# The opening of an attention and two-MoE kernel: one product on GpSimd, the bonus pairs on ScalarE's queue, the way back in another order

## The reference

```python
for t in range(S):                                   # attention
    cur = einsum('bhd,bhe->bhde', u * k[t], v[t])    # bonus of the own step
    y[t] = einsum('bhd,bhde->bhe', r[t], state + cur)
    state = w * state + einsum('bhd,bhe->bhde', k[t], v[t])
h = x @ w_in                                         # dense layer
g = where(h > 0, h, exp(min(h, 0)) - 1)
x = g @ w_out
# experts: argmax of x @ w_gate, relu(x @ w1[e]) @ w2[e] times the gate, 384 slots each
```

## Time and profile before

| | us |
|---|---|
| median of 3 runs | 416.25 |
| lowest and highest | 415.97, 416.66 |
| profiled execution, device time | 416.52 |
| its span in the trace | 414.7 |
| TensorE busy | 406.5 (98%) |
| VectorE busy | 242.7 (59%) |
| GpSimd busy | 231.8 (56%) |
| ScalarE busy | 188.4 (45%) |

### The profile page before, as it was taken

One profiled execution on the slowest core, in us unless ns is written; L12 is line 12 of the kernel. 1 busy time (PEld: TensorE's weight loads), 2 busy tenths in 40 slices (PEclk: granted clock), 3 DMA queues, 4 the chain that ended last, 5 costly groups with the idle time before them and its releaser, 6 DMA issues.

```text
span 414.7 us, 9451 instructions
## 1 busy us (share of the span) xinstructions
PE 406.5 (98%) x3697; PEld 390.2 (94%) x3697; DVE 242.7 (59%) x576; ACT 188.4 (45%) x409; POOL 231.8 (56%) x239
## 2 busy tenths in 40 slices
PE   8999999999999999999999999999999999999994
PEld 8799799999999999999999999999999999999994
DVE  7787955375576547654754487775645546365421
ACT  4786543233433333333333555553645446464420
POOL 3789865467856685668234336075174461835531
PEclk9999999999999999999999999999999999999999
DMA  7999996204030403020018001827283844729000
GB/s 261 403 395 365 350 366 245 91 29 155 4 119 2 138 21 118 3 85 21 2 21 342 2 2 39 324 77 256 116 321 101 326 169 193 295 90 357 5 31 28
DMA packets 18650, 64.98 MB, mean 157 GB/s; under 512 B 2203, under 2 KB 11717, under 8 KB 16432
## 3 DMA queue, kind: packets, MB, share of 16 engines
q1 hardware_dynamic: 16816, 59.68, 39.5%
q0 software_dynamic: 1792, 4.73, 3.0%
HBM read 51.98 MB, written 13.21 MB: 157 GB/s over the span
## 4 chain that ended last, share of the span: by engine, by line
PE 89%; DVE 4%; DMA 3%; issue 1%; POOL 1%; ACT 1%; POOLq 0%; SPq 0%; DVEq 0%
PE bank L1362 26%; PE bank L1364 25%; PE bank L1363 25%; PE bank L1383 2%; DMA xrow<-slots 2%; PE bank L1412 1%; PE bank L1448 1%; PE bank L1452 1%; PE bank L1686 1%; PE bank L1441 1%; PE bank L1444 1%; PE bank L1539 1%; PE bank L1721 1%; PE bank L1722 1%; PE bank L1625 1%
## 5 line engine op out<-in xcount | busy, mean ns | idle before, releaser
L708 POOL TENSOR_TENSOR g_lo<-elu,g_hi 128x256 fp32r<-128x256 f32 x95 | 74.0, 780 | 86.3 <-ACT g_hi L875 85.7
L1362 PE MATMUL bank<-xt,wd_hi 128*128 128x256 f32 x285 | 80.5, 283 | 0.6 <-DVE elu L1190 0.6
L1364 PE MATMUL bank<-xt,wd_lo 128*128 128x256 f32 x285 | 80.4, 282 | 0.0
L1363 PE MATMUL bank<-xt,wd_hi 128*128 128x256 f32 x285 | 80.3, 282 | 0.0
L866 ACT ACTIVATE elu<-elu 128x256 f32<-128x256 f32 x96 | 40.1, 418 | 76.4 <-DVE elu L1182 75.9
L1362 PE MATMUL bank<-wd_hi,g_hi 128*128 128x392 f32 (+1 forms) x192 | 67.4, 351 | 0.0
L1364 PE MATMUL bank<-wd_hi,g_lo 128*128 128x392 f32 (+1 forms) x192 | 65.2, 340 | 0.0
L1363 PE MATMUL bank<-wd_lo,g_hi 128*128 128x392 f32 (+1 forms) x192 | 65.1, 339 | 0.0
L1190 DVE SCALAR_TENSOR_TENSOR elu<-elu,bank 128x256 f32<-128x256 f32 x96 | 40.3, 420 | 41.1 <-ACT elu L866 41.1
L875 ACT CAST g_hi<-elu 128x256 fp32r<-128x256 f32 x96 | 39.0, 406 | 44.0 <-DVE elu L1190 44.0
L1362 PEld LDWEIGHTS bank<-xt,wd_hi 128*128 128x128 f32 x285 | 53.9, 189 | 1.3 <-DVE elu L1190 1.1
(11 more groups left out here) (220 smaller groups left out, 945.1 us busy)
## 6 DMA issues: line engine op xcount, KB each, us to landing
we_raw<-wexp SPq DMA_DIRECT2D x8, 1536.0 KB, 7.9
wd_raw<-wexp SPq DMA_DIRECT2D x8, 1536.0 KB, 8.9
rkt<-rkt SPq DMA_DIRECT2D x12, 512.0 KB, 5.8
nat<-nat SPq DMA_DIRECT2D x9, 672.0 KB, 5.1
xrow<-slots SPq DMA_DIRECT2D x16, 193.0 KB, 7.4
wd_raw<-win SPq DMA_DIRECT2D x4, 768.0 KB, 9.3
wd_raw<-wout SPq DMA_DIRECT2D x4, 768.0 KB, 9.7
wo_tr<-wouttr SPq DMA_DIRECT2D x1, 3072.0 KB, 18.6
```

What stands on the lines that cost most here:

```text
L708: nc.gpsimd.tensor_tensor(g_lo[:, f % 4, :], elu[:, f % 2, :], g_hi[:, f % 4, :].bitcast(F32), ALU.subtract).then_inc(s_glo, 1)
L1362: mm(dst, w_hi, x_hi, start=start, stop=False)
L1363: mm(dst, w_hi, x_lo, start=False, stop=False)
L1364: return mm(dst, w_lo, x_hi, start=False, stop=stop)
```

## The change

The raw product of chunk 0 is made by GpSimd, as soon as `rkt` of chunk 0 is there, and no more by VectorE. VectorE in turn makes the second half of chunk 0's diagonal, by one multiply of the unit matrix with `bon` (new semaphore `s_half0`), in place of four activations of ScalarE. The load of the bonus pairs is issued by ScalarE ahead of its first work, not by SP between the two `rkt` loads. On GpSimd the diagonal of chunk 1 comes ahead of the natural keys of chunk 0. On TensorE the bonus sums of chunk 1 come ahead of the scores of chunk 0, the way back of chunk 0 ahead of its outer products, and in the way back of chunk 1 the part from the state comes last and alone waits for it. ScalarE splits x of chunk 0 ahead of copying the state. For chunks after the first two, the bonus sums are made with 4 repetitions of the pair instead of 32 (only chunk 2 uses that).

```diff
             sp.dma_start(w4[:, :], decay).then_inc(s_par, 16)
             load_rkt(0)
-            sp.dma_start(u_pair[:, :, :], bonus_pair).then_inc(s_up, 16)
             load_rkt(1)
...
+            pool.wait_ge(s_rkt[0], 16)
+            nc.gpsimd.tensor_tensor(rk_pair(0), rkt[0][:, 0, :, :], rkt[0][:, 1, :, :], ALU.mult).then_inc(s_prod, 1)
             diagonal(0)
+            diagonal(1)
             pool.wait_ge(s_k1, 2)
             natural_k1(0)
-            diagonal(1)
             natural_k1(1)
...
+            nc.scalar.dma_start(u_pair[:, :, :], bonus_pair).then_inc(s_up, 16)
             act.wait_ge(s_const, NPOOLC)
...
-            half_diagonal(0)
             bonus_copy(1)
             half_diagonal(1)
             w_in_hi(0)
+            x_hi(0)
             act.wait_ge(s_u, 1)
             nc.scalar.copy(z[1][:, :, :], u_bank(0).rearrange("p (h e) -> p h e", h=HP)).then_inc(s_z, 1)
-            x_hi(0)
             w_in_hi(1)
...
-                if c < 2 and j == 1:
-                    dve.wait_ge(s_half, c + 1)
+                if c == 0 and j == 1:
+                    dve.wait_ge(s_half0, 1)
+                elif c == 1 and j == 1:
+                    dve.wait_ge(s_half, 1)
...
-            raw_pair(0)
             queries(0)
             keys(0)
+            dve.wait_ge(s_prod, 1)
             raw_pair(1)
             queries(1)
             keys(1)
+            dve.wait_ge(s_bon, 1)
+            dve.wait_ge(s_const, NPOOLC)
+            V.tensor_tensor(att[0][:, 1, :, :], bc(ident[:, :].unsqueeze(1), [128, HP, C]),
+                            bc(bon[0][:, :].rearrange("s (h j) -> s j h", j=2)[:, 1, :].unsqueeze(2), [128, HP, C]),
+                            ALU.mult).then_inc(s_half0, 1)
...
                     pe.wait_ge(s_pwn, 1)
-                    wait_if(pe, s_z, c)
...
                 old = has_state(c)
-                if old:
+                state_first = old and c > 1
+
+                def from_state():
                     for hp in range(HP):
                         for j in range(2):
                             rows = slice(64 * j, 64 * j + 64)
-                            mm(dst(2 * j, hp), z[p][rows, hp, 0:MAIN], r1[p][rows, hp, :], start=True, stop=False,
-                               skip_group_check=True)
+                            mm(dst(2 * j, hp), z[p][rows, hp, 0:MAIN], r1[p][rows, hp, :], start=state_first,
+                               stop=not state_first, skip_group_check=True)
...
+                if not ends:
+                    pe.wait_ge(s_z, n_states(c))
+                    last = from_state()
                 last.then_inc(s_y, 1)
...
             def bonus_sums(c):
+                width = C // 4 if c < 2 else 4
...
+            bonus_sums(1)
             scores(0)
-            bonus_sums(1)
             scores(1)
+            back(0)
             outer(0)
-            back(0)
             back(1)
             outer(1)
```

More of the change, by code:

```diff
@@ L219, in build @@
         s_half = sem("half_diagonal_ready")
+        s_half0 = sem("half_diagonal0_by_dve")
         s_pre = pair("diagonal_ready")
@@ L1440, in back @@
                             rows = slice(64 * j, 64 * j + 64)
-                            mm(dst(2 * j, hp), z[p][rows, hp, 0:MAIN], r1[p][rows, hp, :], start=True, stop=False,
-                               skip_group_check=True)
+                            mm(dst(2 * j, hp), z[p][rows, hp, 0:MAIN], r1[p][rows, hp, :], start=state_first,
+                               stop=not state_first, skip_group_check=True)
                     for hp in range(HP):
-                        mm(dst(1, hp), z[p][:, hp, MAIN:2 * MAIN], r1[p][:, hp, :], start=False, stop=False,
+                        end = mm(dst(1, hp), z[p][:, hp, MAIN:2 * MAIN], r1[p][:, hp, :], start=False,
+                                 stop=not state_first, skip_group_check=True)
+                    return end
+                if state_first:
+                    from_state()
+                ends = state_first or not old
+                for j in range(2):
+                    for hp in range(HP):
+                        mm(dst(2 * j, hp), v_cols(c, hp, j)[0], att[p][:, j, hp, :], start=not state_first, stop=ends,
                            skip_group_check=True)
@@ L1447, in back @@
                     for hp in range(HP):
[L1448 to L1452, removed]
+                        last = mm(dst(1, hp), v_cols(c, hp, j)[1], att[p][:, j, hp, :], start=False, stop=ends and j == 1,
                                   skip_group_check=True)
+                if not ends:
+                    pe.wait_ge(s_z, n_states(c))
+                    last = from_state()
                 last.then_inc(s_y, 1)
             def bonus_sums(c):
+                width = C // 4 if c < 2 else 4
                 pe.wait_ge(s_up, 16)
@@ L1459, in bonus_sums @@
                 for hp in range(HP):
-                    last = mm(bonus_bank(c)[:, hp, :, :], rk_pair(c)[:, hp, :], bc(u_pair[:, hp, :].unsqueeze(1), [128, C // 4, 2]),
+                    last = mm(bonus_bank(c)[:, hp, 0:width, :], rk_pair(c)[:, hp, :], bc(u_pair[:, hp, :].unsqueeze(1), [128, width, 2]),
                               start=True, stop=True)
```

## The result

The changed kernel takes 416.66 us (median of 20 runs, 415.93 to 417.32) against 415.94 for the kernel before (20 runs on the same chip, 415.54 to 416.66). The ratio is 1.0016, 95% interval 1.0010 to 1.0022: about 0.7 us slower. The interval leaves out 1, but the difference is under the 0.2% that the prediction took as the least that can be told apart. The profiled execution of after took 416.26, with a span of 414.4; that of before had taken 416.52. So the two profiled executions stand the other way round than the medians, and single places in them must be read, not their totals.

The account below looks back on a forecast made before the run. TensorE is 98% busy, so the start of its steady work, set by the end of VectorE's masks, bounds. Masks 1.0 later (+0.60 +0.60 +0.55 −0.72) gave 417.5, less 0.27 to the median, 417.2; range 415.7 to 417.9.

Parts of the forecast that it names:

- rival 4: Opening 1.0 later, but slack before 38 us, most likely in GpSimd's waits, gives it back: 416.3 to 416.9; chance 0.12.
- The bound: TensorE is 98% busy; an edit of the opening is worth only how much it moves the steady work's start.
- GpSimd's product holds the doubling: Opening: GpSimd's multiply makes VectorE's last doubling wait, 1.1 later on the powers, against 0.60 saved.
- Rivals 1 and 2: Product costs VectorE nothing: 416.3, chance 0.16; or diagonal 1 also early or side by side: 415.2 to 415.7, chance 0.14.
- rival 3: Natural keys of chunk 0 on GpSimd also pass ahead of VectorE's new multiply, 1.14 more: 418.4; chance 0.08.
- The half diagonal: VectorE's new multiply in the opening: 0.60 of work, 0.55 waiting for GpSimd's diagonal 1, ending at 11.6.
- x_hi(0) ahead of the state copy costs nothing on ScalarE, which is waiting there: ScalarE in the opening: splitting x of chunk 0 before copying the state costs nothing.
- hold back no mask: TensorE's scores, now behind the bonus sums, are done at 10.9 and 12.0 and delay none of VectorE's masks.
- One to one: What moves the end of the opening's masks moves everything after, nearly one to one; masks forecast 1.0 later.
- The load of the bonus pairs: 4 KB load ahead of ScalarE's table load: over well before its scalings at 5.76; SP's later loads issued about 0.45 sooner.
- The narrow sums: TensorE's sums of chunk 2, 8 columns instead of 64: 0 to 0.2 saved, 0 at the end.

Follow-up runs that it names:

- b_delay: The kernel before with a memset of 1024 columns on VectorE ahead of the last mask, result unused; 417.29 us, ratio 1.0029 to before.
- a_neither: The changed kernel with chunk 0's raw product back on VectorE and the second half of diagonal 0 back on ScalarE; 416.63 us, ratio 1.0012 to before.
- a_half_act: The changed kernel with only the second half of chunk 0's diagonal back on ScalarE; 416.99 us, ratio 1.0022 to before.
- c_sums: a_neither with the scores of chunk 0 again ahead of the bonus sums of chunk 1 on TensorE; 416.54 us, ratio 1.0004 to before.
- b_cast: The kernel before with the VectorE copy of `n_seen` at 84 us written as a sum over one element; 415.68 us, ratio 0.9984 to before.
- b_prod: The kernel before with only the raw product of chunk 0 moved to GpSimd; 416.68 us, ratio 1.0014 to before.
- b_half: The kernel before with only the second half of chunk 0's diagonal moved from ScalarE to VectorE; 416.83 us, ratio 1.0015 to before.
- b_cast_up: b_cast with the bonus pairs also loaded through ScalarE's queue, as in the changed kernel; 415.60 us, ratio 0.9983 to before.

## Why the prediction was right, and where it was not

The forecast of 417.2 stood 0.5 above the median, which lies inside the range. Some 0.3 of the 0.5 is the base: the prediction started from 416.25, the median of three runs, and the 20 runs beside the changed kernel gave 415.94. As a difference 1.0 was forecast and 0.7 measured, inside the band of 0.6 to 1.3; as a time 416.66 lies just under that band's 416.8, and inside the 416.3 to 416.9 of rival 4. So the time alone doesn't tell the forecast from rival 4; the traces of the opening do, as far as 38 us. Step by step:

- **The bound was right.** What counts is when the steady work starts: b_delay, where a memset of 0.91 and a load 0.2 late delayed the masks, moved the outer products by 1.20 and the time by 1.2 us.
- **GpSimd's product holds the doubling: right, with its numbers.** 1.5 was forecast for the held step, 1.49 measured; w_end 6.84 and 6.71; end of the keys 10.4 and 10.33. Rivals 1 and 2, which needed the product to be free, fell with that row; rival 3 fell with the masks at 11.28, ahead of the end of the natural keys.
- **The half diagonal: right mechanism, smaller size.** Forecast were 0.6 of work and 0.55 of waiting, with the end at 11.6. GpSimd's select came at 10.17 instead of 10.4 and so overlapped VectorE's keys for longer; the multiply was over at 11.36. Masks: end 13.88, not 14.2, 0.73 later and not 1.0.
- **"x_hi(0) ahead of the state copy costs nothing on ScalarE, which is waiting there": this step failed.** ScalarE waits before x, not behind it. The state copy left the wait and went between x and the rounding of w_in, which the second splits and all of GpSimd's chunk 2 wait for: 0.3 in after, and most of the 0.44 in a_neither. TensorE's new order, with the outer product behind the way back of chunk 0, has its part in it: the outer product ends at 14.38, so the copy could no longer run in the wait before x. The sum had no term for the instructions queued behind the copy.
- **The scores behind the bonus sums "hold back no mask": true in after**, since the new multiply stood ahead of the mask. In a_neither and in a_half_act they hold the first mask by 0.80, and c_sums shows what that order costs: 0.18 of the 0.55.
- **The two misses cancelled.** The outer products of chunk 2 were forecast at 39.2 and stood at 39.39: 0.3 too much on VectorE, 0.3 to 0.4 too little on ScalarE. The right number at 38 us is no proof of the sum.
- **"One to one" to the end: half right.** The 1.17 of the profile is measured as 0.7. Rival 4 had the loss given back, but sought it in GpSimd's waits before 38 us. In the profile of after it was given back behind them: 0.59 with the copy of `n_seen`, 0.39 at 97 us, 0.40 at 385 us. Whether the copy is held can't be read from the recorded starts, which are 0.02 to 0.03 apart in the same order in all profiles. That a shifted opening decides it anew is argued and not shown. b_cast shows what is at stake: 0.7 us. How often the copy is held in before and in after can't be told from one profile each. The two b_ kernels whose profiles also have the short copy, b_prod and b_half, still came out at 1.0014 and 1.0015, and like after they have wide spreads (416.03 to 417.16, 416.00 to 417.45); but so has c_sums (415.60 to 417.14), with the long copy. This part stays open.
- **The load of the bonus pairs was priced at nothing, from a profile in which the next load happened to be early.** With that load late, the opening of before is 0.2 to 0.7 later in other executions, and the distance of after from it that much shorter. b_cast_up didn't show a gain from it in the median, so its share in 0.7 against 1.17 is open too.
- **The narrow sums: right.** 8 matmuls with 8 columns follow one another from 21.86 to 22.66, first start to last; with 64 columns it was 20.62 to 21.45, 0.03 more.

## What to carry to other kernels

Before work is moved from VectorE to GpSimd, look at what VectorE does with two SBUF inputs in the time that the GpSimd instruction takes: the saving of 0.60 brought a wait of 1.07, and the wait was nearly as long for a 4-column step (0.94). When an instruction is moved out of an idle time of an engine, ask who is queued behind its new place; an idle time ahead of an instruction says nothing about the time behind it. And where small fp32 copies on VectorE run beside GpSimd multiplies, writing them as one-element reductions may be worth a trial: here one such edit gave 0.16%, as much as the whole change had cost.

## What the runs showed of the hardware

- A VectorE copy with one SBUF input and 8 columns a partition took 0.74 in nine profiles, beside a GpSimd multiply of 0.74 that had started 0.02 to 0.03 ahead, and 0.16 in three others with 0.02 between the starts. A reduction over the same data took 0.14 both times.
- A GpSimd memset of 128x1024 (0.95) held no two-input step of VectorE; a GpSimd multiply of 128x512 held one by 1.07 and another by 0.94.
- A 4 KB load with small packets on the same queue ahead of a load of `rkt` (two halves of 128x512 fp32): from issue to landing 5.4 to 5.8 in six profiles of seven, against 4.5 to 4.8 with that small load on another queue.
- Matmuls with 128x128 fp32 weights follow one another at 0.11 to 0.12 with 8 columns (0.80 from the first start of eight to the last) and with 64 (0.83).
- A load of rows at 375 us took 9.0 to 9.6 from issue to landing in the fourteen profiles.
